# Two blocks of a first feed-forward layer moved into the product groups of the second

## The reference

```python
# gated linear attention, per head
state = f[t] * state + outer(k[t], v[t]);  y[t] = q[t] @ state
x = y as [3072 tokens, 384]
# first feed-forward layer, d_ff = 1536
x = ((x @ w_a) * (x @ w_b)) @ w_out
# second one: 4 experts, d_ff = 1024 each
p = domain_probs / (domain_probs.sum(-1) + 1e-9)
out = sum over e of p[:, e] * (max(x @ w1[e], 0) @ w2[e])
```

## Time and profile before

| | |
|---|---|
| time, median of 3 runs | 1312.23 us (1311.81 to 1313.07) |
| span of the profiled execution | 1310.4 us |
| median less that span (launch and end around it) | 1.8 us |
| TensorE busy | 1301.5 us, 99% |
| VectorE, ScalarE, GpSimd busy | 825.4, 622.0, 549.4 us |
| share of TensorE in the chain that ended last | 97% |

### The profile page before, as it was taken

The page is one execution under the profiler, slowest core; times in us unless marked ns, Lnnn a source line. Parts: engine busy times, 40 slices in busy tenths (PEclk is TensorE's granted clock), DMA queues, the critical chain, the costliest instruction groups (busy, mean ns, idle before and its releaser), DMA issues.

```text
span 1310.4 us, 23459 instructions
## 1 busy us (share of the span) xinstructions
PE 1301.5 (99%) x8223; PEld 1278.5 (98%) x8223; DVE 825.4 (63%) x1678; ACT 622.0 (47%) x1259; POOL 549.4 (42%) x560
## 2 busy tenths in 40 slices
PE   8999999999999999999999999999999999999998
PEld 7999999999999999999999999999999999999998
DVE  7855554555433324367777777777677776777765
ACT  7654544444432323354545554545544455544442
POOL 3321211212135856234445644446544447444441
PEclk9999999999999999999999999999999999999999
DMA  8512122122204343132332343322343313343211
GB/s 253 157 59 60 54 62 60 53 62 61 62 1 144 99 140 125 31 97 80 96 97 72 91 136 91 89 91 69 107 125 96 95 63 93 98 131 98 87 60 49
DMA packets 71686, 117.59 MB, mean 90 GB/s; under 512 B 7120, under 2 KB 49808, under 8 KB 71568
## 3 DMA queue, kind: packets, MB, share of 16 engines
q1 hardware_dynamic: 71568, 116.08, 29.4%
HBM read 102.94 MB, written 14.55 MB: 90 GB/s over the span
## 4 chain that ended last, share of the span: by engine, by line
PE 97%; DVE 1%; DMA 1%; SPq 0%; issue 0%; ACT 0%; DVEq 0%
PE bank L1885 12%; PE bank L1887 11%; PE bank L1886 11%; PE bank L2119 10%; PE bank L2120 10%; PE bank L2121 10%; PE bank L2013 8%; PE bank L2015 8%; PE bank L2014 8%; PE bank L1829 2%; PE bank L1880 2%; PE bank L1868 1%; PE bank L2091 1%; PE bank L2090 1%; PE bank L2089 1%; PE bank L1812 1%
## 5 line engine op out<-in xcount | busy, mean ns | idle before, releaser
L1270 POOL TENSOR_TENSOR wu<-w_r,wu 128x640 fp32r<-128x640 f32 (+1 forms) x132 | 200.6, 1522 | 315.1 <-ACT wu L954 315.1
L2119 PE MATMUL bank<-wd,h_hi 128*128 128x384 f32 x768 | 259.8, 338 | 0.5 <-issue 0.3
L2120 PE MATMUL bank<-wd,h_hi 128*128 128x384 f32 x768 | 257.6, 335 | 0.0
L2121 PE MATMUL bank<-wd,h_lo 128*128 128x384 f32 x768 | 257.1, 335 | 0.0
L1678 DVE SCALAR_TENSOR_TENSOR xt<-bank,pn,xt 128x384 f32<-128x384 f32 x288 | 177.2, 615 | 101.0 <-PE bank L2121 91.7
L981 ACT ACTIVATE h_hi<-h 128x384 fp32r<-128x384 f32 x240 | 124.6, 524 | 193.4 <-DVE h L1628 81.5
L2015 PE MATMUL bank<-x_lo,wu 128*128 128x384 f32 x600 | 202.6, 338 | 0.0
L2013 PE MATMUL bank<-x_hi,wu 128*128 128x384 f32 x600 | 201.4, 336 | 0.0
L2014 PE MATMUL bank<-x_hi,wu 128*128 128x384 f32 x600 | 200.8, 335 | 0.0
L1885 PE MATMUL bank<-xs_hi,wab 128*128 128x384 f32 x570 | 196.8, 345 | 1.4 <-ACT a_sb L992 1.4
L1886 PE MATMUL bank<-xs_hi,wab 128*128 128x384 f32 x570 | 191.2, 335 | 0.0
(11 more groups left out here) (158 smaller groups left out, 2406.2 us busy)
## 6 DMA issues: line engine op xcount, KB each, us to landing
w_r<-weight_sums SPq DMA_DIRECT2D x120, 320.0 KB, 2.9
raw<-w SPq DMA_DIRECT2D x48, 576.0 KB, 3.9
unit<-fkq SPq DMA_DIRECT2D x28, 504.0 KB, 4.2
v_in<-v_chunks SPq DMA_DIRECT2D x32, 144.0 KB, 3.9
out<-xt SPq DMA_DIRECT2D x24, 192.0 KB, 4.4
weight_sums<-w_s SPq DMA_DIRECT2D x10, 384.0 KB, 4.4
weight_sums<-w SPq DMA_DIRECT2D x40, 64.0 KB, 2.7
raw<-w SPq DMA_DIRECT2D x6, 384.0 KB, 3.2
```

What stands on the lines that cost most here:

```text
L1270: eng.tensor_tensor(wu_piece(g, n, 1), wu_raw(g, n), wu_piece(g, n, 0).bitcast(f32), ALU.subtract).then_inc(s_ulo, 1)
L2119: eng.matmul(o, hh, w_hi, start=(f == fs[0]), stop=False)
L2120: eng.matmul(o, hh, w_lo, start=False, stop=False)
L2121: mm = eng.matmul(o, hl, w_hi, start=False, stop=(f == fs[-1]))
```

## The change

Blocks 6 and 7 of the first layer leave the loop over steps j, which now ends at j = 216 (`PLAIN = 6`). They become a pass of eight groups ahead of the four passes of the second layer. A pair of groups covers three f tiles: the first makes a with w_a (15 products, result in `h2`), the second b with w_b (15 products, result in the new `hb`). GpSimd multiplies the two (`product`, six times 128x384), ScalarE rounds, VectorE writes the rest (`h1_rest`), and the down products of a pair (six tiles of 9 matmuls) are laid into the two groups behind it, three in each. VectorE adds the tiles to the block's place in `xt`.

The weights of these eight groups need sums as well: 18 groups of sums now, made from j = 31, one for each 9 steps, beside the attention. `w_s` has one buffer instead of two. The small group of each pass of the second layer now comes first instead of last, and the order in which x is split at a pass's start follows.

The diff, cut to its core:

```diff
--- before.py
+++ after.py
...
+    PLAIN = 6
+    N1 = PLAIN * FT1
     TB = 512
     NP = NB1 // 2
     FG = 3
     NQ = E * FT2 // FG
     LAST = E * FT2 - FG * NQ
-    GP = NQ + 1
-    G = NP * GP
+    NF = FT1 // FG
+    PASSES = [(1, b) for b in range(PLAIN // 2, NP)] + [(2, b) for b in range(NP)]
+    GROUPS = [(p, q) for p, (ffn, _) in enumerate(PASSES) for q in (range(2 * NF) if ffn == 1 else (NQ, *range(NQ)))]
+    G = len(GROUPS)
+    NS = 2 * NF + NQ
...
-    X_NEXT = (8, 14, 1, 9, 2, 7, 12, 11, 5, 10, 6, 13, 3, B21, 4, 0, B10)
+    X_SUMS = (1, 2, 5, 9, 7, 6, 8, 14, 12, 11, 10), (8, 14, 1, 9, 2, 7, 12, 11, 5, 10, 6)
+    X_PLAIN = (13, 3, 4, 0), (B21, B10, 13, 3, 4, 0)
...
-    SUMS_AT, SUMS_PACE = CMIN_AT, 8
-    WU_AT, WD_AT = (3 * FT1 * (NB1 - 1) + 18, 3 * FT1 * (NB1 - 1) + 32), 3 * FT1 * (NB1 - 1) + 29
+    SUMS_AT, SUMS_PACE = 31, 9
+    WU_AT, WD_AT = (3 * FT1 * (PLAIN - 1) + 18, 3 * FT1 * (PLAIN - 1) + 32), 3 * FT1 * (PLAIN - 1) + 29
 
     def x2_at(n):
-        return SUMS_AT + 4 + 8 * n if n < 8 else 3 * FT1 * (NB1 - 1) + 2 + 2 * (n - 8)
+        return CMIN_AT + 9 + 2 * n
...
+        w_s = sb(perm, "w_s", [128, len(W_SUMS), 128])
+        plain = ExitStack()
+        a_sb = sb(plain, "a_sb", [128, TB1])
+        h_sb = sb(plain, "h_sb", [128, TB1])
+        h_hi = sb(plain, "h_hi", [128, 2, TB1], f32r)
+        h_lo = sb(plain, "h_lo", [128, 2, TB1], f32r)
+        plain.close()
+        hb = sb(perm, "hb", [128, 2 * FG, TB1])
...
+        def makes_a(g):
+            return ffn(g) == 1 and q_of(g) % 2 == 0
+
+        def makes_h(g):
+            return not makes_a(g)
+
+        def full(g):
+            return ffn(g) == 1 or q_of(g) < NQ
+
+        def sums_of(g):
+            return q_of(g) if ffn(g) == 1 else 2 * NF + q_of(g)
...
+        def dest(g):
+            return h2 if makes_a(g) or ffn(g) == 2 else hb
+
+
+        def acc_1(g, n):
+            return x_tile(2 * blocks_of(g) + T_ORDER[n] // KT, T_ORDER[n] % KT)
...
+                if q < 2 * NF:
+                    f0, width = q // 2 * FG * 128, FG * 128
+                    eng.dma_start(dst, (wa, wb)[q % 2][:, f0:f0 + width].rearrange("(k p) f -> p k f", p=128))\
+                       .then_inc(s_wr, 16)
+                    return
...
-                    sums_stored(eng)
-                    eng.wait_ge(s_wcp, 16 * 4 * NQ)
+                    attention_done(eng)
                 else:
                     eng.wait_ge(s_uhi, 3 * (g - 1) + n + 1)
                     eng.wait_ge(s_ulo, 3 * (g - 1) + n + 1)
-                b, q = group(g)
-                if q < NQ:
+                if full(g):
+                    q = sums_of(g)
+                    sums_stored(eng, q)
+                    eng.wait_ge(s_wcp, 16 * 4 * (q + 1))
                     src = wsum[q, :, n * WP:(n + 1) * WP, :]
...
+            def h1_round(g, n):
+                o = H_ORDER[n]
+                eng.wait_ge(s_mul, products(g) + n + 1)
+                h2_free(g)
+                eng.activation(h2_hi[:, half(g), o, :], hb[:, o, :], ACT.Copy).then_inc(s_h2hi, 1)
...
+                elif ffn(g) == 1:
+                    copy(g, 0)
+                    copy(g, 1)
+                    up_round(g + 1, 0)
+                    if nxt:
+                        sum_hi(nxt, 0)
+                        sum_hi(nxt, 1)
+                    copy(g, 2)
+                    h1_round(g, 0)
+                    up_round(g + 1, 1)
+                    if nxt:
+                        plain_hi(nxt, 2)
+                        sum_hi(nxt, 2)
+                    copy(g, 3)
+                    copy(g, 4)
+                    up_round(g + 1, 2)
+                    if nxt:
+                        plain_hi(nxt, 3)
+                        sum_hi(nxt, 3)
+                    h1_round(g, 1)
+                    h1_round(g, 2)
+                    if nxt:
+                        plain_hi(nxt, 4)
+                        sum_hi(nxt, 4)
+                    h1_round(g, 3)
+                    h1_round(g, 4)
+                    if nxt:
+                        plain_hi(nxt, 5)
+                        sum_hi(nxt, 5)
...
+            def product(g, n):
+                o = H_ORDER[n]
+                eng.wait_ge(s_add, adds(g) + (3, 6, 7, 8, 9, 10)[n])
+                eng.tensor_tensor(hb[:, o, :], h2[:, o, :], hb[:, o, :], ALU.mult).then_inc(s_mul, 1)
...
+            for g in range(1, G):
+                p, q = GROUPS[g]
+                nxt = p + 1 if g == final_of(p) and g + 1 < G else None
+                if ffn(g) == 1 and makes_a(g):
+                    for n in range(3):
                         up_rest(g + 1, n)
-                    if change:
-                        x2_rest(change, 2 * n)
-                        x2_rest(change, 2 * n + 1)
-                if g:
-                    for n in range(len(f_tiles(g % GP))):
+                    for n in range(FG):
+                        down_rest(g + 1, n)
+                elif ffn(g) == 1:
+                    up_rest(g + 1, 0)
+                    if nxt:
+                        sum_lo(nxt, 0)
+                        sum_lo(nxt, 1)
+                    product(g, 0)
+                    up_rest(g + 1, 1)
+                    if nxt:
+                        sum_lo(nxt, 2)
+                    up_rest(g + 1, 2)
+                    product(g, 1)
+                    product(g, 2)
+                    product(g, 3)
+                    product(g, 4)
+                    product(g, 5)
...
+            def h1_rest(g, n):
+                o = H_ORDER[n]
+                eng.wait_ge(s_h2hi, results(g) + n + 1)
+                eng.tensor_tensor(h2_lo[:, half(g), o, :], hb[:, o, :], h2_hi[:, half(g), o, :].bitcast(f32),
+                                  ALU.subtract).then_inc(s_h2lo, 1)
...
+                if ffn(g) == 1:
+                    d, to = tile_bank(g, n), acc_1(g, n)
+                    if q_of(g) == 1 and n == 0:
+                        x_used(GROUPS[g][0])
+                    eng.wait_ge(s_tile, tiles(g) + n + 1)
+                    if q_of(g) == 1:
+                        eng.tensor_copy(to, d).then_inc(s_acc, 1)
+                    else:
+                        eng.wait_ge(s_acc, tiles(g - 2) + n + 1)
+                        eng.tensor_tensor(to, to, d, ALU.add).then_inc(s_acc, 1)
+                    return
...
+                elif ffn(g) == 1:
+                    add(g, 1)
+                    add(g, 2)
+                    add(g, 3)
+                    if q > 1:
+                        weigh(g - 2, 3)
+                    h1_rest(g, 0)
+                    add(g, 4)
+                    if nxt:
+                        plain_lo(nxt, 2)
+                    add(g, 5)
+                    add(g, 6)
+                    if q > 1:
+                        weigh(g - 2, 4)
+                    add(g, 7)
+                    add(g, 8)
+                    h1_rest(g, 1)
+                    if nxt:
+                        plain_lo(nxt, 3)
+                    add(g, 9)
+                    add(g, 10)
+                    h1_rest(g, 2)
+                    if nxt:
+                        plain_lo(nxt, 4)
+                    h1_rest(g, 3)
+                    if q > 1:
+                        weigh(g - 2, 5)
+                    h1_rest(g, 4)
+                    if nxt:
+                        plain_lo(nxt, 5)
+                    h1_rest(g, 5)
+                elif full(g):
+                    add(g, 1)
+                    add(g, 2)
+                    weigh(g - 1, 0)
+                    add(g, 3)
+                    h2_rest(g, 0)
...
-                        down_2(g - 1, n)
-                    elif n == 4:
-                        down_1(N1 - 1)
+                    if g == 0:
+                        if n == 4:
+                            down_1(N1 - 1)
+                    elif ffn(g) == 2:
+                        down(g - 1, n)
+                    elif makes_a(g):
+                        if n % 2 == 0:
+                            down(g - 1, n // 2)
+                    elif q_of(g) > 1:
+                        if n % 2 == 1:
+                            down(g - 2, 3 + n // 2)
             for n in range(TT):
-                down_2(G - 1, n)
+                down(G - 1, n)
```

More of the change, by code:

```diff
@@ L505, in results, with products, parts @@
+        def products(g):
+            return sum(2 * FG if ffn(x) == 1 and makes_h(x) else 0 for x in range(g))
         def results(g):
-            return sum(2 * len(f_tiles(x % GP)) for x in range(g))
+            return sum(2 * len(fs_of(x)) for x in range(g) if makes_h(x))
+        def parts(g):
+            return len(shares(q_of(g))) if ffn(g) == 2 else 1
         def tiles(g):
-            return sum(TT * len(shares(x)) for x in range(g))
+            return sum(TT * parts(x) for x in range(g) if makes_h(x))
@@ L511, in w_downs, with downs, down_group, half @@
         def w_downs(g):
-            return sum(len(f_tiles(x % GP)) for x in range(g))
```

(23 more changed lines are left out.)

562 lines of the change are left out of this document (324 added, 238 removed).

## The result

| | before | changed |
|---|---|---|
| median | 1312.02 us (1311.49 to 1313.07, 4 runs) | 1343.24 us (1342.35 to 1344.06, 4 runs) |
| ratio to before | | 1.0234 (95% interval 1.0220 to 1.0247) |
| span of the profiled execution | 1310.4 us | 1340.5 us |

A forecast was written before the change was run, and what follows sets the result against it. TensorE was taken to bound the kernel: matmuls times 0.174 us plus its waits. 1310.4 - 12.5 (matmuls) + 22.6 (new groups) + 0.5 (attention) = 1321.0 us; with 1.8 for the median, 1322 was forecast, range 1305 to 1330.

The forecast's parts named there:

- The ledger of the new groups: Engine queues laid side by side for the eight new groups: TensorE waits there of 22.6 us in all.
- a middle b group: In each of two such groups TensorE waits 0.28 us at the fifth product and 0.52 at the tenth.
- the 0.8 or more that was named as a sign: In the new groups, VectorE's `h1_rest` would show a mean of 0.8 us or more in the new profile.
- The attention's sums: Sums for 18 groups beside the attention fit GpSimd's idle time: 0.5 us added, from 0 to 10.
- Costed at nothing: Weights' way over DRAM and the second layer's new order: no cost, bounds -2 to +3 us for the lot.
- No turns: Rival: in the new groups GpSimd and VectorE don't hold each other; 11.9 us of waits, 1312 us, chance 0.18.
- The turns: In the new groups, GpSimd's multiplications and VectorE's rests exclude each other when they meet; included in the 22.6 us.
- Slower by more: Rival: sums beside the attention delay gates or unit loads, adding 5 to 18 us: 1327 to 1340, chance 0.14.
- the rule that I cited: VectorE instructions with two SBUF inputs and GpSimd ones reading SBUF lock each other out; with at most one, not.

The follow-up runs named there:

- experiment 1: Changed kernel with GpSimd's three down-weight rests ahead of the fifth rest of x, in each second-layer pass's last full group: 1327.06 us.
- Experiment 2: Changed kernel with 94 extra matmuls, results overwritten, filling TensorE's longest waits ahead of the first down tile at four places: 1336.23 us.
- experiment 3: Changed kernel with VectorE's `h1_rest` reading one SBUF operand instead of two, the subtraction of the high part left out: 1336.68 us.
- experiment 6: As experiment 1, but VectorE makes the 24 products of a and b, GpSimd keeping only its weight rests: 1326.97 us.
- experiment 7: As experiment 1, same instructions, new order on TensorE, ScalarE, VectorE and GpSimd from the attention's end: 1304.68 us; with TensorE's order kept, 1310.82 us.
- 4: As experiment 3, but the one operand is read as 192 elements, each twice, against the changed kernel: 1336.89 us.
- experiment 5: Changed kernel with ScalarE's copies ahead of its first rounding in each b group, and VectorE's first rest behind its fifth addition: 1342.91 us.

## Why the prediction was wrong

**What held.** TensorE bounds, and time is matmuls at 0.174 us plus its waits. The ledger of the new groups, 22.6 us, came out at 20.9, at the places that it named: 0.36 and 0.40 us in a middle b group (forecast 0.28 and 0.52), 1.79 and 1.43 behind it (1.65 and 1.6), 4.25 at the next pass (4.2). The one place that is off is behind the first b group, 2.3 us for 4.0; there the half speed filled a wait, as said below, and experiment 1, without it, has 1.70 and 2.21 us. The product was priced at 1.02 us and takes 1.01 to 1.02 undisturbed, with a mean of 1.12; the rests have the 0.8 or more that was named as a sign. The attention's sums cost nothing, as most of that term's argument said.

**The step that failed: "Costed at nothing".** It said that in the second layer "work per pass is equal; x's roundings go into groups where ScalarE and GpSimd were half idle", bounds -2 to +3. It came to 19.2 us. Half idle was an average; what counts is the place. The small group behind a pass's last full one has only 9 matmuls ahead of its first down tile, and the rests of the down weights that this tile needs stand last in GpSimd's queue, behind a rest of x that waits for ScalarE. I ran the ledger only over the groups with new instructions. Run over this place as well, after the result, and with TensorE's wait for those rests put in, it gives 4.4 us and 0.1 for each start; measured are 4.6. Experiment 1 shows the cause: one change of order takes 16.2 us.

**What was missing: the clock.** I took the granted clock of the kernel before, 1.00 throughout, for a constant. Behind each wait over 4 us, and behind some of about 2, it falls to the lower level, and TensorE's work is nearly twice as long until it rises again: 1.2 to 2.7 us each time. Experiment 2 shows the link. This is 9.6 us of the sum, though not all of it is loss: in experiment 1 the first pair had no half-speed stretch at 463 us, and a wait of 1.70 us at 470 us that the changed kernel doesn't have. Matmuls at half speed there ran in time that TensorE would have waited anyway. (Experiment 1 has 1.5 us at half speed later in that pair instead, from 476 us on.)

**The rivals.** "No turns" predicted that without them the waits halve. The turns exist, and experiment 3 takes a part away and gains 6.6 us. But experiment 6 takes most of them away with all of GpSimd's products and gains nothing, and experiment 7 keeps them (rests 0.96 us) and gains 22. The turns lengthen a chain where the order has left no slack. I had argued that GpSimd, with 11 of 12.6 us in a b group, is the limit; a pair has 25 us for its 18.7, and the limit was how soon its last products were wanted. "Slower by more" (1327 to 1340) came nearest in time, but by a mechanism that the trace doesn't show: the attention ends no later than before.

A word on the rule that I cited. The Trainium skill (SBUF — State Buffer, "Who interferes with whom") has an instruction with one SBUF input free of contention only outside the modes that use two ports, and names `tensor_scalar` among those that can enter one. I left that condition out. The 2.32 us of experiment 3 agree with the page, not with my short form of it.

## What to carry to other kernels

A change of order has to be followed to every wait of the bounding engine for what was moved past it, in the stretches called equal too; an engine's busy share says nothing of when its last result is wanted. A wait of TensorE of over 4 us has to be priced with the matmuls at half speed behind it, and one of about 2 us may have to be, unless these only fill another wait. When a saving of work vanishes into waits while no helper is full (VectorE 72%, GpSimd 68% of 458 to 564 us), order is the first suspect: 16 us in experiment 1 and 22 more in experiment 7 came back here with the same instructions, and the change then makes the kernel 0.56% faster. That is 7.3 us of the 12.5 that the matmuls promised.

## What the hardware showed

- The clock falls behind single waits: in the changed kernel and experiments 1, 3, 4, 5 and 6 it did so behind all 16 waits of 4.2 to 4.9 us. From the matmul that waited or up to 0.65 us behind it, 8 to 18 matmuls start 0.32 us apart, then 0.17 again. Behind waits of 2.0 to 2.2 us it was seen at some places and not at others. Behind waits of 1.3 to 2.0 us close together it was seen in experiment 5 (2.1 and 1.2 us, both middle pairs) and experiment 6 (1.2 us), and at the same places not in the changed kernel nor in experiment 1.
- VectorE's `tensor_scalar` from SBUF to SBUF takes 0.34 to 0.36 us for 128x384 in float32, where `tensor_tensor` takes 0.54 to 0.56, also when its operand is read with each element twice. While GpSimd multiplies it is held as the longer one is: 1.16 us each in a pair, for 1.35.
